# Windowed attention with sinks and two feed-forward layers: plain float32 products in place of split ones for the values and for the first batch's scores

## The chip, the cores and the metric

The kernel runs on one core of one Trainium2 chip. TensorE multiplies, VectorE (DVE), ScalarE (ACT) and GpSimd (POOL) work element by element, and SyncE (SP) issues nearly all transfers. The metric is device time in microseconds, the median of several executions: 657.28 us before the change (three runs, 656.28 to 657.93).

## What is computed

Attention for 2 batches, 8 heads, 768 positions and a head size of 64. A query sees its own and the 127 positions before it, and the first 4 positions (the sinks). Then come two feed-forward layers of 1536 tokens, model width 512 and hidden width 2048. All inputs and outputs are float32.

```python
scores = q @ k.T / sqrt(64)                      # masked to window 128 and 4 sinks
a = exp(scores - max); a = a / (sum(a) + 1e-9)
x = (a @ v).transpose(0, 2, 1, 3).reshape(1536, 512)
h = x @ w_in;   g = maximum(0.01 * h, h);  x = g @ w_out     # layer 1
h = x @ w2_in;  g = h * sigmoid(h);        y = g @ w2_out    # layer 2
```

## The kernel before

Each engine's program is written out by hand. All of them run over the same steps `a = 0..51` (`LAST = NPAIR + 4`). The queries are cut into 12 tiles `T` of 128 positions (6 to a batch); a tile has 4 pairs of heads, so that pair `u = 4T + p` is one of 48 and head `n` one of 96. Step `a` works on the scores of the next pair, the softmax of pair `a`, the transposes of pair `a-1` and the value products of pair `a-2`. A half `e` is two pairs: 4 heads of one tile.

The first `FS = 19` steps, called the head here, hold attention alone. From `a = 19` on each step also does one step `F = a - 19` of layer 1: `hidden(F+1)` (L1095, 12 products of 512 columns) and `project(F)` (L1112, another 12). Layer 1 has 48 such steps in three blocks of 512 tokens. `hidden(0)` needs `x` of tiles 0 to 3, so it waits for half 7. After attention, layer 1 runs on by itself, and then layer 2, whose first product is done by Strassen's scheme (`strassen`, L1139).

Every float32 operand of a matrix product is split in two parts of type fp32r: ACT writes the high part (a copy with a cast), and DVE or POOL writes the low part (the operand less the high part). A product then takes several passes of fp32r:

- Scores (`scores`, L1021): `q_st` holds the high part of q in partitions 0 to 63 and the low part in 64 to 127, `k_hl` the two parts of k, each in both halves of the partitions. Two passes of 260 columns (128 in the first tile of a batch) give a head's scores. ACT makes the high parts in `high_qk` (L548, two instructions for half a tile), POOL the low ones in `low_qk` (L434). So that both halves of the partitions have the data, `load_qk` (L321) loads it twice: 2 x 260 KB for half a tile.
- Values (`weigh_values`, L1062): stationary are 128 columns of v (two heads), moving are 256 columns of turned probabilities (two heads of 128 queries). For each of one or two key tiles three passes are run (`PASSES`). `high_v` (ACT, L559) and `low_v` (POOL, L456) split v; `high_pair` (ACT, L565) and `low_pair` (DVE, L761) copy the turned probabilities out of PSUM in two parts.
- The transposes of the probabilities (`turn_pair`, L1032) and of the inverse sums (`turn_half`, L1045), and the sink products (`weigh_sinks`, L1083).

In the head TensorE also runs filler products on zeros (`fill`, L1015): 24 ahead of everything, 3 in each of the steps 0 to 7, and 1 in each of the others. They give nothing to the result. The scores of the head go round three PSUM banks (`s_bank`), the transposes round two.

DVE's work for a step stands in this order: mask and maximum of two heads (`mask_max`, L748), `low_pair`, the sums' inverses, `take_half` or `scale_half` (L768, L796), then the low parts of first-layer weights (`low_win` L805, `low_wout` L811). SP issues in program order and waits in it: loads of q and k, of v, and from `a = 9` on the weights (`first_loads`, then `load_ws`).

Of the kernel before, what the change touches and what calls it, by code (L numbers as in the profile page):

```python
# [12 lines left out]
P = 128  # L13
# [4 lines left out]
def sink_window_attention_two_ffn(  # L18
    nc: bass.Bass, qk: bass.AP, vt: bass.AP, vsink: bass.AP, w1: bass.AP, w2: bass.AP, out: bass.AP,
    n_sink: int, window: int, seq: int,  # L20
):
    TILES, _, D, _, _ = qk.shape
    HD = vt.shape[2]
# [15 lines left out]
    NB = TILES // TB  # L39
    assert D == 64 and HD == 512 and REP == 4 and window <= P and NS <= P and FT == 16 and TILES == 12 and TPB == 6  # L40

    KEPT = 6
    RING = 4
    QR = 3

# [87 lines left out]
    with ExitStack() as ctx:  # L133
# [12 lines left out]
        w7_even_low = sb("w7_even_low", [P, 7, 2 * P], F32R)  # L146

# [9 lines left out]
        v_raw = sb("v_raw", [P, HD], F32)  # L157
        q_st = sb("q_st", [P, H, P], F32R)
        k_hl = sb("k_hl", [P, 2, H, PAN], F32R)
        v_hl = sb("v_hl", [P, 2, 2, HD], F32R)  # L160
# [17 lines left out]
        pT = sb("pT", [P, 2, 2, 512], F32R)  # L178
# [7 lines left out]
        def over(at, *tensors):  # L186
# [13 lines left out]
        (xs_even, w7_odd, w_sums, x_sums, w7_even_high), end = over(  # L200
            att_at, ("xs_even", [7, 2, BLK], F32R), ("w7_odd", [2, 7, 2 * P], F32R), ("w_sums", [2, 5, 2 * P], F32),
            ("x_sums", [2, 2 * P], F32), ("w7_even_high", [7, 2 * P], F32R))
# [18 lines left out]
        def o_bank(e):  # L221
            return y_ps[3] if e < E_EARLY and e % 2 else o_ps

# [32 lines left out]
        v_loaded = sem("v_loaded")  # L256
# [7 lines left out]
        v_high, v_ready = sem("v_high"), sem("v_ready")  # L264
# [8 lines left out]
        t_written, t_high, t_ready = sem("t_written"), sem("t_high"), sem("t_ready")  # L273
# [27 lines left out]
        def j_split(T):  # L301
            return 1 if T < TB else 3 if T == TB else 2

        split_1 = {(T, 3): T + 1 for T in range(TB)}
        split_1.update({(T, 0): T for T in range(TB + 1, TILES)})
# [14 lines left out]
        def _(sp):  # L320
            def load_qk(T, half):  # L321
                c = 2 * T + half
                wait(sp, k_ready, c - QR + 1)
                wait(sp, q_ready, c - QR + 1)
                for lo in (0, D):
                    sp.dma_start(qk_raw[lo:lo + D, c % QR, :, :], qk[T, half]).then_inc(qk_loaded[c % QR], 16)

            def load_v(T):
                wait(sp, v_ready, 2 * T)
                sp.dma_start(v_raw[:, :], vt[T]).then_inc(v_loaded, 16)  # L330
# [42 lines left out]
            load_qk(0, 0)  # L373
            load_qk(0, 1)
            load_v(0)
            load_qk(1, 0)
            for a in range(LAST):
                T, j = divmod(a, PAIRS)
                if j == 0 and T + 1 < TILES:
                    load_qk(T + 1, 1)  # L380
                if j == 2 and T + 1 < TILES:
                    load_v(T + 1)
                if j == 2 and T + 2 < TILES:
# [921 lines left out]
```

## Time and profile before

| | us |
|---|---|
| median of 3 runs | 657.28 |
| the profiled execution | 657.99 |
| its span, first to last instruction | 656.1 |
| `hidden(0)` begins (end of the head) | 65.2 |
| PE busy / DVE busy / ACT busy / POOL busy | 629.0 / 390.9 / 348.1 / 148.8 |

PE is TensorE's products, PEld its weight loads, which run beside the products. Rows of the time line merge neighbouring instructions of one kind, so a row's time covers all of its count; products overlap at their ends, so that the time from one to the next is less than the duration of one. In tables, "idle before" is the time that an engine stood still just before these instructions, and what ended it.

### The profile page before, as it was taken

How to read it: one execution, taken by the hardware profiler on the slowest of the kernel's cores; microseconds unless marked ns; L12 is line 12 of the kernel's file. 1: busy time of each engine (PE TensorE's matmuls, PEld its weight loads, DVE VectorE, ACT ScalarE, POOL GpSimd, SP SyncE). 2: the span in 40 equal slices, each digit the busy share in tenths (PEclk: the TensorE clock that was granted, in tenths of full speed). 3: DMA queues.
4: the chain of work that ended last, by engine and by line, in shares of the span. 5: the costliest groups of instructions: out<-in, count | busy, mean ns of one | idle time of the engine just before them, and what ended most of it. 6: DMA issues, size and time to landing. Idle time of an engine off the chain costs nothing.

```text
span 656.1 us, 10261 instructions
## 1 busy us (share of the span) xinstructions
PE 629.0 (96%) x3523; PEld 535.5 (82%) x3523; DVE 390.9 (60%) x812; ACT 348.1 (53%) x755; POOL 148.8 (23%) x181
## 2 busy tenths in 40 slices
PE   8896999989989999999999999999999999999997
PEld 4676787777878888888787888999998999999896
DVE  3887456555534656653157646676767677665652
ACT  6696656555545566642145446464655546454532
POOL 6775414232214323310418600000000000000000
PEclk9998999999999999999999999999999999999999
DMA  6666233334321232121148754434444543445401
GB/s 150 170 159 199 74 113 98 119 112 125 97 82 33 80 98 81 66 93 32 77 126 289 255 173 150 156 112 153 135 131 144 199 162 114 153 131 198 136 1 65
DMA packets 26611, 82.72 MB, mean 126 GB/s; under 512 B 3520, under 2 KB 3520, under 8 KB 26560
## 3 DMA queue, kind: packets, MB, share of 16 engines
q1 hardware_dynamic: 26176, 82.00, 39.7%
q8 instruction: 29, 0.48, 0.3%
q14 instruction: 22, 0.18, 0.1%
q10 hardware_dynamic: 384, 0.07, 0.1%
HBM read 73.66 MB, written 8.39 MB: 125 GB/s over the span
## 4 chain that ended last, share of the span: by engine, by line
PE 77%; DVE 9%; ACT 5%; issue 5%; POOL 1%; ACTq 0%; DVEq 0%; POOLq 0%
PE y_ps L1181 20%; PE h_ps L1106 18%; PE y_ps L1126 14%; PE s_ps L1134 8%; PE h_ps L1134 8%; PE t_ps L1134 3%; PE o_ps L1074 3%; DVE win L808 2%; DVE wout L814 2%; ACT prob L544 2%; PE t_ps L1042 1%; DVE g L819 1%; PE s_ps L1029 1%; ACT wout L587 1%; DVE att L802 1%
## 5 line engine op out<-in xcount | busy, mean ns | idle before, releaser
L1106 PE MATMUL h_ps<-x,win 128*128 128x512 f32 x576 | 144.7, 396 | 9.1 <-DVE win L808 5.2
L1126 PE MATMUL y_ps<-g,wout 128*128 128x512 f32 x576 | 146.9, 395 | 1.2 <-PE o_ps L1074 1.2
L1181 PE MATMUL y_ps<-wout,g 128*128 128x512 f32 x576 | 139.7, 391 | 0.0
L1106 PEld LDWEIGHTS h_ps<-x,win 128*128 128x128 f32 x576 | 104.7, 188 | 32.2 <-DVE win L808 6.9
L1181 PEld LDWEIGHTS y_ps<-wout,g 128*128 128x128 f32 x576 | 104.8, 188 | 20.4 <-issue 0.4
L1126 PEld LDWEIGHTS y_ps<-g,wout 128*128 128x128 f32 x576 | 103.6, 188 | 21.1 <-issue 2.3
L814 DVE TENSOR_TENSOR wout<-w_raw,wout 128x512 fp32r<-128x512 f32 x84 | 61.8, 736 | 59.4 <-ACT wout L587 59.4
L544 ACT ACTIVATE prob<-sm,neg_max 128x260 f32<-128x260 f32 (+1 forms) x96 | 47.0, 490 | 53.7 <-DVE neg_max L757 53.7
L593 ACT ACTIVATE g_f<-h_ps 128x512 f32<-128x512 f32 x48 | 28.6, 595 | 75.5 <-PE h_ps L1106 75.4
L650 ACT ACTIVATE g_f<-c_sum 128x512 f32<-128x512 f32 x24 | 15.2, 632 | 83.5 <-DVE c_sum L872 83.5
L819 DVE TENSOR_TENSOR g<-g_f,g 128x512 fp32r<-128x512 f32 x48 | 35.1, 732 | 30.1 <-ACT g L595 30.1
L587 ACT ACTIVATE wout<-w_raw 128x512 fp32r<-128x512 f32 x84 | 50.0, 623 | 0.0
L757 DVE CUSTOM_DVE_ANT_0 sm<-s_ps,mask 128x260 f32<-128x260 f32 (+1 forms) x71 | 28.7, 404 | 34.7 <-PE s_ps L1029 34.1
L461 POOL TENSOR_TENSOR v_hl<-v_raw,v_hl 128x256 fp32r<-128x256 f32 x24 | 20.4, 850 | 105.1 <-ACT v_hl L563 105.0
L879 DVE TENSOR_TENSOR g<-g_f,g 128x512 fp32r<-128x512 f32 x48 | 33.0, 687 | 17.6 <-ACT g L639 16.3
L446 POOL TENSOR_TENSOR q_st<-qk_raw,q_st 64x512 fp32r<-64x512 f32 x24 | 30.8, 1284 | 39.5 <-ACT q_st L555 37.9
L1134 PE MATMUL s_ps<-xs_even,w_odd 128*128 128x256 f32 x288 | 38.3, 282 | 0.0
L1134 PEld LDWEIGHTS s_ps<-xs_even,w_odd 128*128 128x128 f32 x288 | 37.2, 191 | 1.2
L1074 PE MATMUL o_ps<-pT,v_hl 128*128 128x256 f32 x222 | 34.6, 290 | 1.0 <-DVE pT L765 0.7
L1134 PE MATMUL h_ps<-xs_even,w_even_high 128*128 128x256 f32 x192 | 35.2, 282 | 0.0
L1029 PEld LDWEIGHTS s_ps<-k_hl,q_st 128*128 128x128 f32 x142 | 26.2, 190 | 9.9 <-issue 4.3
L1029 PE MATMUL s_ps<-k_hl,q_st 128*128 128x260 f32 (+1 forms) x142 | 29.8, 292 | 3.7 <-DVE neg_max L757 3.7
(133 smaller groups left out, 1017.3 us busy)
## 6 DMA issues: line engine op xcount, KB each, us to landing
w_sums<-w_sums SPq DMA_DIRECT2D x32, 640.0 KB, 3.9
w_raw<-w SPq DMA_DIRECT2D x36, 512.0 KB, 3.3
w_raw<-w SPq DMA_DIRECT2D x48, 384.0 KB, 3.0
qk_raw<-qk SPq DMA_DIRECT2D x48, 260.0 KB, 4.6
stage<-w SPq DMA_DIRECT2D x8, 512.0 KB, 5.3
v_raw<-vt SPq DMA_DIRECT2D x12, 256.0 KB, 2.9
y<-qk_raw SPq DMA_DIRECT2D x12, 256.0 KB, 3.8
vs_raw<-vsink ACTq DMA_DIRECT2D x8, 8.0 KB, 4.9
```

Of the source, the lines that this page charges most:

```text
L446: nc.gpsimd.tensor_tensor(q_low, qk_raw[D:P, c % QR, :, 0:P], q_low.bitcast(F32), ALU.subtract).then_inc(q_ready, 1)
L544: nc.scalar.activation(prob[:, n % PR, 0:W], sm[:, n % 2, 0:W], ACT.Exp, scale=-1.0, bias=neg_max[:, n % 4:n % 4 + 1], accum_out=row_sum[: ...
L587: nc.scalar.activation(wout[:, split_slot[j], 0, :], w_raw[:, j % RING, HD:2 * HD], ACT.Copy).then_inc(wout_high, 1)
L814: nc.vector.tensor_tensor(wout[:, slot, 1, :], w_raw[:, j % RING, HD:2 * HD], wout[:, slot, 0, :].bitcast(F32), ALU.subtract).then_inc(wou ...
L819: nc.vector.tensor_tensor(g[:, 1, F % 2, :], g_f32[:, F % 2, :], g[:, 0, F % 2, :].bitcast(F32), ALU.subtract).then_inc(g_ready, 1)
L879: nc.vector.tensor_tensor(g2[:, q % 2, 1, part, :], g_f32[:, half, :].rearrange("p (i n) -> p i n", i=2), g2[:, q % 2, 0, part, :].bitcast ...
L1029: ins = mm(bank_[:, 0:W], q_st[:, h, :], k_hl[:, part, h, 0:W], start=part == HI, stop=part == LO)
L1074: ins = mm(pair_out(u), v_hl[:, s, vp, p * P:(p + 1) * P], pT[:, u % 2, pp, s * 2 * P:(s + 1) * 2 * P], start=(u % 2 == 0 and s == 0 and v ...
L1106: ins = mm(h_ps[:, :], win[:, split_slot[split_of[F]], wp, c * P:(c + 1) * P], x[:, xp, c, tokens(F)], start=(c == 0 and wp == HI and xp = ...
L1126: ins = mm(y_ps[d][:, :], wout[:, split_slot[split_of[F]], wp, d * P:(d + 1) * P], g[:, gp, F % 2, :], start=(first and wp == HI and gp == ...
L1134: ins = mm(to, w_part(q, w_i, 1, wp)[:, 0, c * P:(c + 1) * P], x_part(q // FP, x_i, xp)[:, c, :], start=start and c == 0 and wp == HI and ...
L1181: ins = mm(y_ps[d][:, :], g2[:, q % 2, gp, at, d % 2 * P:(d % 2 + 1) * P], wout[:, slot, wp, :], start=(first and wp == HI and gp == HI), ...
```

## The change

- All value products (`weigh_values`) use v as loaded and the turned probabilities as copied, both plain float32, in one product for each key tile. `high_v`, `low_v` and `low_pair` go; `high_pair` becomes `take_pair`, one copy into a float32 `pT`. v has a ring of four tiles (`VR = 4`).
- The first batch's scores (tiles 0 to 5, `PLAIN = 6`) use q and k as loaded, in plain float32. Heads lie in partitions 0 to 63 or 64 to 127 (from a new input `qk_first`), and each tile is loaded once. A head's product contracts over 64 rows; outside the first tile it is two products, one of 132 and one of 128 columns (or 128 and 132), because the previous tile's keys are read where they were loaded. In the head the two heads of a pair alternate, product by product. `high_qk` and `low_qk` are left for tiles 6 to 11 only, at steps given by `split_0` and `split_1`.
- Filler: 6 in place of 24 at the start, and 1 in each step in place of 3 in the first eight.
- SP's order of loads follows this. Waits that counted pairs and halves together (`t_ready`) are now two semaphores. `w7_even_high` gets room of its own.

```diff
+            def load_plain(T):
+                wait(sp, s_written, H * (T - QR + 2) if T >= QR else 0)
+                raw = qk_raw[:, T % QR, :, :]
+                if T == 0:
+                    sp.dma_start(raw[:, 0:1, :], qk_first[T, :, 0:1, :]).then_inc(first_loaded, 16)
+                    sp.dma_start(raw[:, 1:, :], qk_first[T, :, 1:, :]).then_inc(plain_loaded[T % QR], 16)
+                else:
+                    sp.dma_start(raw, qk_first[T]).then_inc(plain_loaded[T % QR], 16)
...
             def load_v(T):
-                wait(sp, v_ready, 2 * T)
-                sp.dma_start(v_raw[:, :], vt[T]).then_inc(v_loaded, 16)
+                wait(sp, pv_done, PAIRS * (T - VR + 2) if T >= VR else 0)
+                sp.dma_start(v[:, T % VR, :], vt[T]).then_inc(v_loaded[T % VR], 16)
...
-                nc.scalar.activation(pT[:, u % 2, 0, 0:n], t_bank(k)[:, 0:n], ACT.Copy).then_inc(t_high, 1)
+                nc.scalar.activation(pT[:, u % 2, 0:n], t_bank(k)[:, 0:n], ACT.Copy).then_inc(pT_ready, 1)
...
-            def low_pair(u):
-                k = job["pair", u]
-                dve.wait_ge(t_high, u + 1)
-                n = 2 * P if width(u // PAIRS) == P else 4 * P
-                nc.vector.tensor_tensor(pT[:, u % 2, 1, 0:n], t_bank(k)[:, 0:n], pT[:, u % 2, 0, 0:n].bitcast(F32),
-                                        ALU.subtract).then_inc(t_ready, 1)
...
+            def plain_scores(heads):
+                T, W = heads[0] // H, width(heads[0] // H)
+                own = qk_raw[:, T % QR, :, :]
+                ahead = qk_raw[:, (T - 1) % QR, :, :]
...
+                for n in heads:
+                    wait(pe, s_read, freed(s_bank, n))
+                if W == P:
+                    parts = ((own, P, 0, P),)
+                elif T % 2:
+                    parts = ((own, P, P, P + NS), (ahead, P, 0, P))
+                else:
+                    parts = ((own, P, 0, P + NS), (ahead, P + NS, P + NS, P))
+                for part, (raw, at, to, size) in enumerate(parts):
+                    for n in heads:
+                        p, rows = n % H // 2, slice(n % 2 * D, (n % 2 + 1) * D)
+                        ins = mm(s_bank(n)[:, to:to + size], own[rows, p, 0:P], raw[rows, p, at:at + size],
+                                 start=part == 0, stop=True, skip_group_check=True)
...
-                    for vp, pp in PASSES:
-                        ins = mm(pair_out(u), v_hl[:, s, vp, p * P:(p + 1) * P],
-                                 pT[:, u % 2, pp, s * 2 * P:(s + 1) * 2 * P],
...
+                    tile = T if T % 2 == s else T - 1
+                    ins = mm(pair_out(u), v[:, tile % VR, p * P:(p + 1) * P],
+                             pT[:, u % 2, s * 2 * P:(s + 1) * 2 * P], start=u % 2 == 0 and s == 0,
+                             stop=only and s == slots[-1], skip_group_check=True)
...
-                        fill(24)
-                    for n in range(2 * a + 2 if a else 0, min(2 * a + 4, 2 * FS)):
-                        scores(n)
+                        fill(6)
+                    for n in range(2 * a + 2 if a else 0, min(2 * a + 4, 2 * FS), 2):
+                        plain_scores((n, n + 1))
...
-                    fill(3 if a < 2 * PAIRS else 1)
+                    fill(1)
```

## Rows read from the trace of the kernel before

**Rows 1.** The page's first part: busy time, share of the span, instructions.
```profile
PE 629.0 (96%) x3523; PEld 535.5 (82%) x3523; DVE 390.9 (60%) x812; ACT 348.1 (53%) x755; POOL 148.8 (23%) x181
```
**Rows 2.** Windows: length, busy (count) by engine, granted clock, DMA share, GB/s.
```profile
2.00:4.00 2.00, 2.00 (x6) 0.64 (x5) 0.00 (x0) 0.00 (x0) 1.77 (x6) 1.00 0.95 254
9.00:48.00 39.00, 33.68 (x224) 26.45 (x224) 32.22 (x117) 32.11 (x101) 30.56 (x35) 1.00 0.62 153
50.00:60.00 10.00, 7.32 (x46) 7.04 (x47) 7.77 (x26) 7.14 (x21) 5.49 (x7) 0.83 0.80 225
100.00:120.00 20.00, 18.97 (x102) 16.04 (x103) 11.55 (x32) 10.14 (x25) 6.61 (x8) 1.00 0.31 100
400.00:500.00 100.00, 100.00 (x632) 90.28 (x631) 69.99 (x111) 54.00 (x97) 0.00 (x0) 1.00 0.41 137
```
**Rows 3.** Time line of the start: start us, us, engine, line, tiles, count.
```profile
0.73 2.47 SPq L326 DMA_DIRECT2D qk_raw<-qk  x4
1.05 8.10 PE L1018 MATMUL y_ps<-filler 128*128 128x512 bf16 x24 [1.05 <-DVE filler L919]
...
5.12 1.28 ACT L555 ACT_TABLE_LOAD   x1 [5.12 <-issue]
...
10.02 0.40 ACT L544 ACTIVATE prob<-sm,neg_max 128x128 f32<-128x128 f32 x1
```
**Rows 4.** Time line of two steps of the head, ACT.
```profile
38.14 0.42 ACT L575 ACTIVATE x<-att 128x256 fp32r<-128x256 f32 x1 [0.59 <-DVE att L802]
38.46 0.58 ACT L570 ACTIVATE pT<-y_ps 128x512 fp32r<-128x512 f32 x1
38.94 0.50 ACT L544 ACTIVATE prob<-sm,neg_max 128x260 f32<-128x260 f32 x1
...
39.93 0.62 ACT L555 ACTIVATE q_st<-qk_raw 128x512 fp32r<-128x512 f32 x1
40.45 0.63 ACT L556 ACTIVATE k_hl<-qk_raw 128x528 fp32r<-128x528 f32 x1
...
41.75 0.42 ACT L563 ACTIVATE v_hl<-v_raw 128x256 fp32r<-128x256 f32 x1 [0.19 <-DMA v_raw<-vt]
...
43.38 0.42 ACT L575 ACTIVATE x<-att 128x256 fp32r<-128x256 f32 x1 [0.23 <-DVE att L802]
```
**Rows 5.** The same stretch, DVE.
```profile
39.07 0.69 DVE L765 TENSOR_TENSOR pT<-y_ps,pT 128x512 fp32r<-128x512 f32 x1 [0.15 <-ACT pT L570]
```
**Rows 6.** Time line of PE in the head.
```profile
19.37 0.82 PE L1018 MATMUL y_ps<-filler 128*128 128x512 bf16 x3
...
45.07 0.66 PE L1042 MATMUL t_ps<-ident,prob 128*128 128x128 f32 x4
...
46.97 0.40 PE L1029 MATMUL h_ps<-k_hl,q_st 128*128 128x260 f32 x2
...
51.03 0.77 PE L1029 MATMUL s_ps<-k_hl,q_st 128*128 128x260 f32 x2 [1.80 <-DVE neg_max L757]
...
65.20 2.97 PE L1106 MATMUL h_ps<-x,win 128*128 128x512 f32 x12 [0.58 <-POOL x L431]
```
**Rows 7.** Time line of PE and PEld in layer 1, beside attention.
```profile
104.22 0.87 PE L1074 MATMUL o_ps<-pT,v_hl 128*128 128x256 f32 x6
...
104.11 0.78 PEld L1074 LDWEIGHTS o_ps<-pT,v_hl 128*128 128x128 f32 x6
```
**Rows 8.** Groups by line and shape, 66 to 250 us: busy, mean ns, idle before.
```profile
L1074 PE MATMUL o_ps<-pT,v_hl 128*128 128x256 f32 x126 | 18.9, 283 | 0.3 <-DVE att L802 0.3
L1029 PEld LDWEIGHTS s_ps<-k_hl,q_st 128*128 128x128 f32 x92 | 17.1, 188 | 4.4 <-issue 0.8
...
L1042 PE MATMUL t_ps<-ident,prob 128*128 128x128 f32 x84 | 12.9, 272 | 0.1
```
**Rows 9.** Waits, 66 to 250 us: total us, times, longest.
```profile
PE h_ps L1106 <- DVE win L808: 5.2, 7, 1.4
```

More of the change, by code:

```diff
@@ L39, in sink_window_attention_two_ffn @@
     NB = TILES // TB
+    PLAIN = TPB
+    assert qk_first.shape[0] == PLAIN and qk.shape[0] == TILES - PLAIN
     assert D == 64 and HD == 512 and REP == 4 and window <= P and NS <= P and FT == 16 and TILES == 12 and TPB == 6
@@ L222, in o_bank, with early @@
             return y_ps[3] if e < E_EARLY and e % 2 else o_ps
+        def early(kind):
+            return sum(1 for (what, _), k in job.items() if what == kind and k < N_EARLY)
         def freed(bank_of, i):
@@ L255, in sink_window_attention_two_ffn @@
         qk_loaded = [sem(f"qk_loaded{i}") for i in range(QR)]
-        v_loaded = sem("v_loaded")
+        plain_loaded = [sem(f"plain_loaded{i}") for i in range(QR)]
+        first_loaded = sem("first_loaded")
+        v_loaded = [sem(f"v_loaded{i}") for i in range(VR)]
         vs_loaded = sem("vs_loaded")
@@ L299, in sunk @@
             return sum(has_sinks(s // 2) for s in range(e))
[L301 to L305, printed above, removed]
+        split_0 = {4 * T - 2: T for T in range(PLAIN, TILES)}
+        split_1 = {4 * T + (T == PLAIN): T for T in range(PLAIN, TILES)}
         CONSTS = 2 + 2 + 2 + 2 + 1 + 2
@@ L557, in high_qk, with take_pair @@
                                      ACT.Copy).then_inc(k_high, 1)
-            def high_v(T, half):
-                act.wait_ge(v_loaded, 16 * (T + 1))
-                wait(act, pv_done, PAIRS * (T - 1) + 2 * (half + 1))
-                part = slice(half * (HD // 2), (half + 1) * (HD // 2))
-                nc.scalar.activation(v_hl[:, T % TPB % 2, 0, part], v_raw[:, part], ACT.Copy).then_inc(v_high, 1)
-            def high_pair(u):
+            def take_pair(u):
                 k = job["pair", u]
@@ L682, in _ @@
                     high_x(scaled_in[a])
[L683 to L686 removed]
+                if a in split_1:
+                    high_qk(split_1[a], 1)
                 if a == FS:
[L688 removed]
                     take_hidden(0)
@@ L1030, in scores, with taken @@
                 ins.then_inc(s_written, 1)
+            def taken(before):
+                k = freed(t_bank, before) - 1
+                if k >= 0:
+                    what, i = list(job)[k]
+                    pe.wait_ge(pT_ready if what == "pair" else half_ready, i + 1)
             def turn_pair(u):
                 k = job["pair", u]
-                wait(pe, t_ready, freed(t_bank, k))
+                taken(k)
                 pe.wait_ge(exp_done, 2 * u + 2)
@@ L1046, in turn_half @@
                 k = job["half", e]
[L1047 removed]
+                taken(k)
                 pe.wait_ge(inv_spread, e + 1)
@@ L1119, in project @@
                         pe.wait_ge(s_read, S_TWO)
-                        pe.wait_ge(t_ready, N_EARLY)
+                        pe.wait_ge(pT_ready, early("pair"))
+                        pe.wait_ge(half_ready, early("half"))
                         pe.wait_ge(att_ready, E_EARLY)
```

149 lines of the change are left out of this document (66 added, 83 removed).

## The prediction

> **What bounds the kernel now.** I read the page's busy times first. PE is busy for 96% of the span [rows 1], so most of the time can only move if PE's work or its few pauses move. The table by windows then splits the span. In layer 2 (400 to 500 us) PE never stops [rows 2]; the change touches nothing there. Between 100 and 120 us, where attention runs inside layer 1, PE is busy 18.97 of 20 us [rows 2]: PE is still the limit, and each added pass costs its whole length. The head, up to the first product of `hidden(0)` at 65.2 us [rows 6], is different. From 9 to 48 us DVE, ACT and POOL are busy 32.2, 32.1 and 30.6 of 39 us, and PE's 33.7 us include fillers [rows 2]. No engine is full, they hand work round in a ring. The time line shows the period: ACT's copy of `x`, once for two steps, comes at 38.14 and 43.38 us [rows 4], so 5.24 us for two steps, 2.62 for one. After 48 us it is slower: 17 us for the last steps, where first-layer weights are split and where PE waited 1.80 us for DVE's maximum [rows 6], with the granted clock at 0.83 of full speed in the ten microseconds that follow (the level of 1.2 GHz for part of them) [rows 2].
>
> So I treat three stretches: the head (65.2 us), attention within layer 1, and the rest (unchanged).
>
> **What goes.** Of DVE: `low_pair`, 0.69 us for a wide pair [rows 5]. For two steps of the head that is 1.4 us, and DVE cannot be full in less than 5.24, so it keeps at most 3.9 us for two steps, 1.9 for one. Of ACT: in four steps it splits two halves of q and k (0.62 + 0.63 each) and two of v (0.42 each) [rows 4], 3.3 us, 0.8 a step. What stays is one copy of 0.58, two exponentials of 0.50 and half a copy of 0.42: 1.8 us. Of POOL: all the splits of q, k and v in the head; it is then no limit. So the element-wise engines would allow about 1.9 us a step in place of 2.62.
>
> The start moves too. Today the first exponential runs at 10.02 us [rows 3], behind two loads of both halves, ACT's two splits and those of DVE and POOL. After the change nothing lies between the load and the scores. ACT issues its own eight small transfers and loads its table until 6.4 us [rows 3], and this does not change, so the first exponential comes at about 6.5 us. Transfers run at 254 GB/s from 2 us on [rows 2], so the first pair of heads (133 KB) and the rest of the tile (400 KB) have landed before about 4.5 us. The six fillers left take 2 to 3 us (24 took 8.1 [rows 3]).
>
> **What PE pays.** No row before shows a plain float32 product that computes (the transposes only move data), so its price must be bounded. Two prices of PE are on record. Streaming: three fillers of 512 columns take 0.82 us, of which one is 0.38 long, so 0.215 us from one to the next [rows 6], or 0.107 for 256 columns. Weight loading: six weight loads of the value products take 0.78 us with 0.188 for a single one [rows 7, 8], so 0.118 from one to the next; that is also the pace of the six products themselves ((0.87 - 0.28) / 5 = 0.118) [rows 7, 8]. The cheapest that a float32 product can be is one pass, 0.118 us for 256 columns. The dearest that follows from the rows is all four products of two parts by two parts, one more than the three passes that the kernel spells out, each with a weight load of its own: 4 x 0.118 = 0.47 us. I take four streams at 0.107, 0.43 us, close to the upper end, because full precision wants the work of the three passes at the least (0.35), and the row nearest in kind is that of those passes.
>
> The Trainium skill, FP8 and Floating Point Precision, section TensorE Precision Notes, says that true float32 is four passes through the array; that would be this same 0.43. The Trainium skill, Perfetto Trace Analysis, section Engine Utilization, halves the output rate for the mode FP32_LOW_HIGH; were that the whole cost, a product would be 0.21 us. No row here shows either.
>
> A score product of 130 columns is by the same count 4 x 0.054 = 0.22 us when streaming sets the pace, and 4 x 0.115 = 0.46 us when every pass loads weights (the two passes of a head take 0.40 us and one is 0.285 long, so they stand 0.115 apart, the pace of weight loads again [rows 6]). The bounds are 0.115 (one pass) and 0.46. I take 0.22, and both ends stay in the range.
>
> **The head, summed.** PE's work up to `hidden(0)`: 38 heads, 8 with one score product and 30 with two, 68 x 0.22 = 15.0; transposes of 18 pairs, 4 x 2 + 14 x 4 = 64 at 0.12 ((0.66 - 0.27) / 3 is 0.13, a little less further on) [rows 6, 8] = 7.7; of 8 halves, 20 x 0.12 = 2.4; value products of 17 pairs, 4 + 13 x 2 = 30 x 0.43 = 12.9; sink products 8 x 0.12 = 1.0; 19 fillers x 0.215 = 4.1. Sum 43.1 us. The two heads of a pair use different halves of the array's rows and different banks. If they ran fully side by side, half of the 15.0 would go: 35.6. I take the middle, 39 us, 2.1 a step, just above what DVE and ACT allow. Ahead of it lie some 6 us (nothing but the first scores can run before the first exponential), and I allow 4.5 us for pauses: the weight splits in the last steps, which remain, and the last chain through DVE, ACT and POOL that `hidden(0)` waits for. That puts `hidden(0)` at 50 us, 15 earlier than now. Transfers do not stop it: up to there five tiles of q, k and v (0.79 MB each), a sixth on its way and four weights of 0.5 MB are about 7 MB, 30 us at 225 to 254 GB/s [rows 2].
>
> **Attention within layer 1.** Here PE is the limit and pays in full. 27 wide pairs: 2 x 0.43 in place of 6 x 0.12, +0.14 each, 3.8 us. Four pairs of tile 6 with one key tile: 0.43 for 0.36, 0.3 us. Ten heads of tiles 4 and 5 still have plain scores, one head at a time: 0.44 in place of 0.22 (two passes 0.115 apart), 2.2 us. Together +6.3. On the other side PE waits seven times, 5.2 us in all, for DVE's low part of `win` [rows 9]. DVE loses 0.69 us a step, which stands ahead of that split in DVE's order, but the wait also runs through ACT, which is not relieved as much in this stretch. I count half, 2.5 us. Net +3.8. The new waits of SP (a free v slot, scores of a tile done before its buffer is loaded again) stand ahead of weight loads in its queue. The one that is latest, for the scores of tile 5 at `a = 24`, is met within the step before, while its data are wanted one to two steps of 5.7 us later; I count nothing for it, and up to 1 us if the cover fails.
>
> Span: 656.1 - 15 + 3.8 = 644.9. The profiled execution took 1.9 us more than its span and lies 0.7 above the median, so **646 us**.
>
> **Rivals.**
> 1. Rows of the array side by side. If the two heads of a pair overlap fully, 3.5 us more go from the head, and with fewer pauses and all of the 5.2 us regained it is 638. For it: different row halves and banks, in alternation. Against: DVE and ACT then bind at 1.9 us a step.
> 2. Emptying the array at each change of shape. Scores contract over 64 rows and everything between them over 128. If PE must finish all before it changes, each change costs the tail of a product: one is 0.28 long at 0.118 apart [rows 7, 8], so some 0.17. Two changes in each of 19 steps are 6.5 us, and 20 in layer 1 3.4 us more: 656, no change worth the name. The Trainium skill, TensorEngine Tiling (Array Packing), section Key Properties, says that changing the tiling mode drains the engine; this speaks against the change, and no row before has a product of 64 rows.
> 3. The other side: every pass loads its weights. A score product then costs 0.46 and a value product 0.47. The head is 43.1 + 68 x 0.24 + 30 x 0.04 = 60.6 us with no overlap, 71 with start and pauses, and layer 1 pays 10 x 0.69 + 27 x 0.23 = 13.1 for 2.5 regained: 656.1 + 6 + 10.6 = 672.7, measured 674. It turns into a loss from about 0.31 us a score product on: there the head gains only 6 us and layer 1 costs as much. Weight loads busy 82% of the span today [rows 1] speak for it; that only 2 parts of a weight exist speaks against it.
> 4. The clock. With 24 fillers cut to 6 and 3 to 1, PE idles after its first scores until the first exponential. Before, a pause of 1.80 us at 51 us [rows 6] stands beside 0.83 of the clock over the next ten [rows 2]. Were the lower level held through the head, streams double: 68 x 0.43 + 30 x 0.86 + 8.2 of filler + the 11 us that loads set = 74 us, `hidden(0)` at 85; with the 3.8 of layer 1 the span is 680, measured 681. It turns into a loss from some 25 us at the lower level.
> 5. The head is shorter but the gain is eaten by the transfers: weights and tiles pulled into a shorter time, as at 50 to 60 us now, with 0.80 of the DMA engines busy [rows 2]. Then `hidden(0)` comes at 58 or so: 654.
>
> **How the numbers follow.** Chances: forecast 0.52 (640 to 652), rival 1 0.14, rival 2 0.12, rival 3 0.10, rival 4 0.05, rival 5 0.07. The range 634 to 660 holds the forecast, rivals 1, 2 and 5, and leaves the two losses of rivals 3 and 4 out, apart from milder forms of them. A measurement of this kernel can tell 0.3% (2 us) from no change. Faster: forecast, rival 1, most of rival 5 and some of rival 2, 0.76. Same: 0.08. Slower: rivals 3 and 4 and a little of 2, 0.16.
>
> **What will show it.** Right: `hidden(0)` near 50 us; first exponential near 6.5; 0.43 us from one value product to the next; PE above DVE in the head; in layer 1 PE busy more and its waits for `win` down; nothing moved from the end of attention on. Wrong: 0.45 us for a score product or weight loads that fill the head (rival 3); gaps around each block of scores (rival 2); a granted clock near half in the head (rival 4); PE waiting for tiles or weights (rival 5). The weakest term is the price of a plain float32 product, for which no row stands.

## The result, and the profile after

The changed kernel takes 653.33 us (median of 5, 652.15 to 654.31) against 657.29 for the kernel before it, run beside it: a ratio of 0.9936, 95% interval [0.9917, 0.9954]. That is 4.0 us less. 11.3 were forecast, so the sign and the range held, and the size did not.

The first lines to set beside [rows 1] and [rows 2]: busy times, then the windows of the same stretches (columns as in [rows 2]).

```profile
PE 632.4 (97%) x3481; PEld 532.4 (82%) x3481; DVE 358.9 (55%) x762; ACT 330.2 (51%) x707; POOL 102.2 (16%) x135
...
9.00:48.00 39.00, 36.88 (x257) 26.68 (x257) 26.53 (x106) 25.81 (x83) 8.77 (x18) 1.00 0.33 113
50.00:60.00 10.00, 8.26 (x50) 6.60 (x50) 4.38 (x18) 4.82 (x15) 1.30 (x3) 1.00 0.24 81
100.00:120.00 20.00, 20.00 (x103) 16.77 (x103) 10.11 (x30) 11.01 (x29) 4.30 (x6) 1.00 0.66 176
400.00:500.00 100.00, 100.00 (x633) 90.53 (x632) 72.49 (x117) 56.11 (x101) 0.00 (x0) 1.00 0.41 135
```

From 9 to 48 us DVE, ACT and POOL fall from 32.2, 32.1 and 30.6 us to 26.5, 25.8 and 8.8, while PE rises from 33.7 to 36.9 of 39. PE is now the bound of the head, as foreseen. The engines that were relieved bring nothing more.

The time line of PE in one whole period of the head (two steps) shows what it does with that time.

```profile
35.01 0.38 PE L1017 MATMUL y_ps<-qk_raw 64*128 64x132 f32 x1
35.02 0.38 PE L1017 MATMUL s_ps<-qk_raw 64*128 64x132 f32 x1
35.23 0.27 PE L1017 MATMUL y_ps<-qk_raw 64*128 64x132 f32 x1
...
35.45 0.27 PE L1017 MATMUL s_ps<-qk_raw 64*128 64x128 f32 x1
35.66 0.66 PE L1054 MATMUL t_ps<-ident,prob 128*128 128x128 f32 x4
36.15 1.03 PE L1086 MATMUL y_ps<-pT,v 128*128 128x256 f32 x4
37.01 0.38 PE L993 MATMUL y_ps<-filler 128*128 128x512 bf16 x1
37.32 0.38 PE L1017 MATMUL h_ps<-qk_raw 64*128 64x132 f32 x1
...
40.22 0.38 PE L1017 MATMUL s_ps<-qk_raw 64*128 64x132 f32 x1
...
50.67 0.35 PE L1017 MATMUL s_ps<-qk_raw 64*128 64x132 f32 x1 [1.57 <-DVE neg_max L751]
...
56.87 3.01 PE L1117 MATMUL h_ps<-x,win 128*128 128x512 f32 x12 [1.07 <-POOL x L458]
```

Three readings. A plain product shows as two records: the four of a wide pair of value products stand (1.03 - 0.38) / 3 = 0.215 us apart, so a product is 0.43 us, the forecast price exactly. The two heads of a pair truly run side by side: their records start 0.01 us apart. And around the block stand gaps. The block's last record begins at 35.45, and the transposes begin 0.21 later, where records inside the block are 0.11 apart; the block's first record, too, is followed only after 0.22. The filler at 37.01 is followed by the scores after 0.31 in place of 0.215. Two steps take 5.21 us (35.01 to 40.22). The 5.24 of [rows 4] is not typical of the kernel before: from the transposes of one half's inverse sums to those of the next it took 4.4 to 7.5 us in the head, 42.6 from half 0 to half 7, where the changed kernel takes 38.3. `hidden(0)` begins at 56.87 us in place of 65.20 [rows 6], 8.3 earlier; 50 was forecast. Of the 8.3, 3.5 are there when half 0 is turned, that is when its inverse sums are transposed (13.04 against 16.52), 4.3 come between half 0 and half 7, and 0.5 after it.

So 8.3 us were gained by the end of the head, and 5.3 are left in the span (656.1 to 650.8). Where the rest went shows in the transposes of the inverse sums, one for each half, in the same place in both programs. In half 8, the first within layer 1, the changed kernel leads by 8.3 us (59.48 against 67.78, by their weight loads), in half 11 by 5.3, in half 19 by 4.8 and in half 23 by 3.9. Three microseconds go within the few steps that still score tiles 4 and 5; one goes slowly from half 19 on, 0.14 a step, the forecast extra cost of a wide pair. Later, between 345 and 360 us, the kernel before loses 1.4 us that the changed one doesn't, 0.92 of it in one pause at 359.58. `one_head` and `early_fill` below have that pause and `changed_again` lacks it, with no difference between their programs there, so I credit it to neither.

### The profile page after: what moved, and what is told of

It reads as the page before. It is cut to its first block, busy times and chain, and to the rows that moved or that the text cites. A ratio compares the mean times of both kernels' runs of the same rounds, so it can differ in the third digit from the quotient of the medians.

```text
span 650.8 us, 9903 instructions
## 1 busy us (share of the span) xinstructions
PE 632.4 (97%) x3481; PEld 532.4 (82%) x3481; DVE 358.9 (55%) x762; ACT 330.2 (51%) x707; POOL 102.2 (16%) x135
## 4 chain that ended last, share of the span: by engine, by line
PE 92%; DVE 3%; issue 2%; ACT 2%; ACTq 1%; POOL 0%; DVEq 0%
PE y_ps L1194 20%; PE h_ps L1117 20%; PE y_ps L1138 19%; PE h_ps L1146 8%; PE s_ps L1146 8%; PE o_ps L1086 5%; PE t_ps L1146 3%; PE t_ps L1054 2%; PE s_ps L1034 1%; PE s_ps L1017 1%; PE t_ps L1064 1%; DVE win L795 1%; ACTq L668 1%; PE y_ps L1086 1%; PE y_ps L1017 1%
## 5 line engine op out<-in xcount | busy, mean ns | idle before, releaser
L1138 PE MATMUL y_ps<-g,wout 128*128 128x512 f32 x576 | 151.6, 403 | 1.2 <-PE o_ps L1086 1.2
L1138 PEld LDWEIGHTS y_ps<-g,wout 128*128 128x128 f32 x576 | 105.6, 188 | 22.9 <-issue 2.7
L801 DVE TENSOR_TENSOR wout<-w_raw,wout 128x512 fp32r<-128x512 f32 x84 | 60.4, 720 | 57.0 <-ACT wout L590 57.0
L1086 PE MATMUL o_ps<-pT,v 128*128 128x256 f32 x148 | 39.7, 388 | 0.3 <-DVE att L789 0.3
L1146 PE MATMUL s_ps<-xs_even,w_odd 128*128 128x256 f32 x288 | 38.3, 282 | 0.0
L449 POOL COPY inv_wide<-row_inv 128x256 f32<-128x256 f32 x24 | 10.0, 417 | 154.6 <-DVE row_inv L781 154.6
L795 DVE TENSOR_TENSOR win<-w_raw,win 128x512 fp32r<-128x512 f32 x36 | 31.4, 871 | 1.4 <-ACT win L584 1.3
L1146 PEld LDWEIGHTS h_ps<-xs_even,w_even_high 128*128 128x128 f32 x192 | 30.3, 188 | 1.6 <-DVE e_sum L853 0.3
L573 ACT ACTIVATE pT<-t_ps 128x512 f32<-128x512 f32 (+1 forms) x40 | 22.5, 562 | 17.4 <-PE t_ps L1054 17.4
```

The costliest lines, as they stand in the source:

```text
L795: nc.vector.tensor_tensor(win[:, slot, 1, :], w_raw[:, j % RING, 0:HD], win[:, slot, 0, :].bitcast(F32), ALU.subtract).then_inc(win_ready, 1)
L801: nc.vector.tensor_tensor(wout[:, slot, 1, :], w_raw[:, j % RING, HD:2 * HD], wout[:, slot, 0, :].bitcast(F32), ALU.subtract).then_inc(wou ...
L1086: ins = mm(pair_out(u), v[:, tile % VR, p * P:(p + 1) * P], pT[:, u % 2, s * 2 * P:(s + 1) * 2 * P], start=u % 2 == 0 and s == 0, stop=onl ...
L1138: ins = mm(y_ps[d][:, :], wout[:, split_slot[split_of[F]], wp, d * P:(d + 1) * P], g[:, gp, F % 2, :], start=(first and wp == HI and gp == ...
L1146: ins = mm(to, w_part(q, w_i, 1, wp)[:, 0, c * P:(c + 1) * P], x_part(q // FP, x_i, xp)[:, c, :], start=start and c == 0 and wp == HI and ...
```

## The experiments

**Each half of the change alone.** `values_only` is the kernel before with the value half; `scores_only` is the changed kernel without it; `old_fills` has both halves and the fillers of before.

```diff
  values_only: scores, their loads and fillers as before
-                    for vp, pp in PASSES:
+                    tile = T if T % 2 == s else T - 1
+                    ins = mm(pair_out(u), v[:, tile % VR, p * P:(p + 1) * P],
+                             pT[:, u % 2, s * 2 * P:(s + 1) * 2 * P], ...)
```

> The kernel before with the value half of the change alone (plain float32 values, one copy of the turned probabilities; scores and fillers as before). Theory A, the head was bound by VectorE's 4.9 us in 5.24: without the low parts it needs 3.5, ScalarE 4.4, GpSimd 3.9 plus its waits, and TensorE 4.6 to 4.7 for two steps. So 4.7 in place of 5.24, hidden(0) at about 61 us; layer 1 costs 0.14 us a step more on TensorE (4.1) and gets 2.5 back; total near 654.5. Theory B, TensorE alone decides everywhere: the head stays, total 3 us slower than before, 660.

It takes 649.28 us against 657.01 for the kernel before beside it, 7.7 us less and more than the whole change brings (ratio 0.9898 [0.9878, 0.9919]). `hidden(0)` begins at 57.39. The same two steps of the head, from the transposes of one half to those of the next but one:

```profile
34.87 0.38 PE L1033 MATMUL t_ps<-ident,inv_wide 128*128 128x128 f32 x2
...
35.20 0.60 PE L1023 MATMUL y_ps<-ident,prob 128*128 128x128 f32 x4
35.63 1.03 PE L1055 MATMUL o_ps<-pT,v 128*128 128x256 f32 x4
36.40 0.50 PE L1071 MATMUL o_ps<-psT,vs_st 128*128 128x256 f32 x2
...
36.78 0.59 PE L1003 MATMUL y_ps<-k_hl,q_st 128*128 128x260 f32 x2
37.21 0.40 PE L1003 MATMUL s_ps<-k_hl,q_st 128*128 128x260 f32 x2
37.45 0.60 PE L1023 MATMUL t_ps<-ident,prob 128*128 128x128 f32 x4
...
39.45 0.38 PE L1033 MATMUL y_ps<-ident,inv_wide 128*128 128x128 f32 x2
```

4.58 us for two steps, with PE again without a pause, against 5.21 with plain scores. Theory A's 4.7 is met, but not its totals: 61 us for `hidden(0)` and 654.5 were expected, because the sum took 5.24 for every two steps of the kernel before, where most took longer. DVE, ACT and POOL are busy for 3.5, 4.3 and 4.0 us of the 4.58. The edit takes splits of v off ACT and POOL along with DVE's low parts, so that it frees the ring as a whole; no run frees DVE alone. From half 8 to half 23 this kernel takes 234.65 us; the kernel before takes 234.10: the float32 values cost 0.55 us there, not 1.6. A wide pair does cost its 0.14 us, but PE stands still for 6.9 us of the stretch in place of 9.2; the waits for `win` among it are 3.8 us in place of the 5.2 of [rows 9]. That layer 1 hides so much of PE's extra work I had counted only in part.

```diff
  scores_only: the changed kernel, with values, weights and their waits as before
-                    ins = mm(pair_out(u), v[:, tile % VR, p * P:(p + 1) * P], ...)
+                    for vp, pp in PASSES:
+                        ins = mm(pair_out(u), v_hl[:, s, vp, p * P:(p + 1) * P],
+                                 pT[:, u % 2, pp, s * 2 * P:(s + 1) * 2 * P], ...)
```

> The changed kernel with the value half undone (values and turned probabilities in two parts again, three passes). Start and fillers as in the changed kernel. Theory A: VectorE has its low parts back and two steps need 5.2 us on it and on TensorE alike, so that the head gains only at its start, hidden(0) at about 61 us; layer 1 pays 0.27 us for the changes of shape and 0.22 us for streaming in each of ten heads, 4 to 5 us, against no gain later on; total near 657. Theory B, splitting q and k was what held the head: hidden(0) at 57 as in the changed kernel, total 652.

653.22 us, ratio 0.9946 [0.9928, 0.9965]; `hidden(0)` at 59.84. Between the two expectations. Two steps take 5.28 us there (33.22 to 38.50), with PE busy for 5.15 and DVE for 4.80: DVE's low parts and PE's plain scores need about the same time. Of the 5.4 us by which `hidden(0)` comes earlier than before, 3.9 are there when half 0 is turned (12.61 us) and 1.5 come between half 0 and half 7; from half 8 to half 23 it loses 2.1 us, not 4 to 5.

```diff
  old_fills: the changed kernel, with
-                        fill(6)
+                        fill(24)
-                    fill(1)
+                    fill(3 if a < 2 * PAIRS else 1)
```

> The changed kernel with the fillers of the kernel before (24, and 3 in each of the first eight steps). The 24 fillers end at 9.1 us, 2.7 us after ScalarE could take the first exponential, and 16 more fillers cost 0.215 us each where TensorE is the bound, 3.4 us; the clock is at its upper level from 6.5 us on, which gave 2.4 us in early_fill. Theory A: hidden(0) at about 56.87 + 2.7 + 2.2 - 2.4 = 59.4 us, total 2 us slower than the changed kernel. Theory B (fillers are free as they were before): hidden(0) at 56 or less.

656.36 us, ratio 0.9997 [0.9986, 1.0008], `hidden(0)` at 59.09: theory A, though not by its own working, since the 24 fillers ended at 7.7 us and not at 9.1 (the clock came up earlier in this execution). These runs together make the sum of the change. The value half brings 7.7 us. The plain scores, added to it with the fillers unchanged, take 7.1 back (649.28 to 656.36). Fewer fillers bring 3.0 (656.36 to 653.33). The kernel before ran beside each group of runs, with medians of 657.0 to 657.6; by the ratios to it the three parts are 6.7, 6.5 and 4.0 us, so each is known to about 1 us. The traces show where they lie:

| us | half 0 is turned at | half 0 to half 7 | half 8 to half 23 |
|---|---|---|---|
| before | 16.5 | 42.6 | 234.1 |
| `values_only` | 15.9 | 36.0 | 234.6 |
| `scores_only` | 12.6 | 41.1 | 236.2 |
| `old_fills` | 13.9 | 39.6 | 238.3 |
| changed | 13.0 | 38.3 | 238.5 |

Plain scores start the head earlier (no split lies between the load and the scores), and cost more in each step after that than the start gives.

**What plain scores cost.** In `full_rows` each score product contracts over all 128 rows, that is over both heads of a pair, so its scores are sums of two heads' and stand for nothing but their time. The heads can't run side by side, and the array's shape never changes.

```diff
-                        p, rows = n % H // 2, slice(n % 2 * D, (n % 2 + 1) * D)
+                        p, rows = n % H // 2, slice(0, P)
```

> The changed kernel with score products that contract over all 128 rows (both heads of a pair at once, so the scores are sums of two heads' and not the reference's). No side by side is possible, but the shape of the array never changes. Theory A, a change of shape costs about 0.16 us: 38 changes in the head go, 6 us, against 7.5 us for the lost overlap, hidden(0) at about 58; and in layer 1 the step from single plain scores gets 0.3 us cheaper per head. If changes of shape cost nothing: hidden(0) at about 64, as with one head after the other.

One execution, 651.89 us, `hidden(0)` at 57.36. Its start is 1.0 us earlier than the changed kernel's (half 0 at 12.06), with part of its first products short; from half 0 to `hidden(0)` it takes 45.3 us against 43.8, the 1.5 more that theory A expects. Two steps of the head:

```profile
34.63 0.46 PE L1017 MATMUL y_ps<-qk_raw 128*128 128x132 f32 x2
34.93 0.39 PE L1017 MATMUL s_ps<-qk_raw 128*128 128x132 f32 x2
35.15 0.38 PE L1017 MATMUL y_ps<-qk_raw 128*128 128x128 f32 x2
35.37 0.39 PE L1017 MATMUL s_ps<-qk_raw 128*128 128x128 f32 x2
35.59 0.60 PE L1054 MATMUL t_ps<-ident,prob 128*128 128x128 f32 x4
...
40.11 0.46 PE L1017 MATMUL s_ps<-qk_raw 128*128 128x132 f32 x2
```

A product of 130 columns is 0.22 us, as forecast. Two steps take 5.48 us, only 0.27 more than the changed kernel, although the overlap, 4 x 0.22 = 0.88 us, is gone. So 0.61 us came back for the four changes of shape that are gone: 0.15 us each. In layer 1 the same shows alone, since a head comes singly there and has no overlap to lose: from half 8 to half 23 `full_rows` takes 235.71 us, the changed kernel 238.46. Nine heads with plain scores lie in between, so 2.75 us is 0.15 for each of their eighteen changes. The Trainium skill, TensorEngine Tiling (Array Packing), section Key Properties, says that a change of tiling mode drains the engine; the trace agrees, with 0.15 us a change here and 0.2 in the single step below.

Within layer 1, the same step of the changed kernel, of `full_rows` and of `values_only` (split scores):

```profile
79.23 1.64 PE L1117 MATMUL h_ps<-x,win 128*128 128x512 f32 x6
80.80 0.71 PE L1017 MATMUL s_ps<-qk_raw 64*128 64x132 f32 x4
81.44 1.13 PE L1086 MATMUL o_ps<-pT,v 128*128 128x256 f32 x4
82.22 1.74 PE L1138 MATMUL y_ps<-g,wout 128*128 128x512 f32 x6
```
```profile
78.46 1.64 PE L1117 MATMUL h_ps<-x,win 128*128 128x512 f32 x6
...
81.06 1.73 PE L1138 MATMUL y_ps<-g,wout 128*128 128x512 f32 x6
```
```profile
78.12 1.64 PE L1086 MATMUL h_ps<-x,win 128*128 128x512 f32 x6
79.59 0.41 PE L1003 MATMUL s_ps<-k_hl,q_st 128*128 128x260 f32 x2
79.84 1.03 PE L1055 MATMUL o_ps<-pT,v 128*128 128x256 f32 x4
80.51 1.73 PE L1107 MATMUL y_ps<-g,wout 128*128 128x512 f32 x6
```

From the start of the six products to that of the value products it is 2.21 us in the first against 1.72 in the last, and to the next six, by which time the second change has been paid as well, 2.99 against 2.39: 0.60 more for one head, of which 0.22 was forecast. `full_rows` needs 2.60. So the two changes of shape are 0.39 of the 0.60, 0.2 each; over the whole stretch shorter waits for `win` give part of that back.

**Side by side or not.** `one_head` issues all products of a head before those of the next.

```diff
-                    for n in range(2 * a + 2 if a else 0, min(2 * a + 4, 2 * FS), 2):
-                        plain_scores((n, n + 1))
+                    for n in range(2 * a + 2 if a else 0, min(2 * a + 4, 2 * FS)):
+                        plain_scores((n,))
```

> The changed kernel with the two heads of a pair one after the other in the head, not product by product in turn. If the two halves of the array's rows truly work side by side, this loses it: a pair of score products of 0.44 us becomes two, 15 steps x 0.44 + 4 x 0.22 = 7.5 us more, hidden(0) at about 64 us. If the records only look simultaneous: hidden(0) stays at 56.9.

One execution, 653.8 us, `hidden(0)` at 56.51: nothing is lost. This does not refute the overlap, since its own time line shows it:

```profile
34.71 0.38 PE L1017 MATMUL y_ps<-qk_raw 64*128 64x132 f32 x1
34.73 0.38 PE L1017 MATMUL s_ps<-qk_raw 64*128 64x132 f32 x1
34.93 0.27 PE L1017 MATMUL y_ps<-qk_raw 64*128 64x132 f32 x1
34.94 0.27 PE L1017 MATMUL s_ps<-qk_raw 64*128 64x132 f32 x1
```

The second head (`s_ps`) starts 0.02 us after the first although it is issued behind all of it. The experiment could not take the overlap away; `full_rows` did.

**The fillers and the clock.** `no_late_fill` drops the fillers from step 4 on; `early_fill` has 3 in steps 0 to 2.

```diff
  no_late_fill
-                    fill(1)
+                    fill(1 if a < 4 else 0)
  early_fill
-                    fill(1)
+                    fill(3 if a < 3 else 1)
```

> The changed kernel without the fillers of steps 4 to 18 (15 of them). Theory A, TensorE is the bound in the head: in the changed kernel two steps take 5.21 us and TensorE has no pause in them, so each filler costs its 0.215 us. Of 15 fillers, two stand just before a pause for a maximum and save nothing; 13 x 0.215 = 2.8 us less, hidden(0) at about 54.1 in place of 56.9 us, total near 650.5. Theory B, the ring through VectorE and ScalarE is the bound and TensorE only looks full: less than 0.5 us of change. A third outcome, the granted clock falls without fillers: later than 56.9.

652.27 us, ratio 0.9924 [0.9907, 0.9942]; `hidden(0)` at 56.19, 0.7 earlier. The scores at 34 to 39 us come about 1 us earlier (4.90 us for two steps in place of 5.21, so some 0.155 for each filler), but the stretch 35 to 57 us then shows 0.92 of the clock, where the changed kernel shows 1.00:

```profile
35.00:57.00 22.00, 18.13 (x119) 14.54 (x118) 13.70 (x51) 14.11 (x41) 4.84 (x12) 0.92 0.25 88
```

Both theory A, at less than its price, and the third outcome are in it. That the missing fillers brought the clock down is likely and not shown: it is one execution of each, and the kernel before, with its fillers, shows 0.92 in the same stretch too.

> The changed kernel with 3 fillers in place of 1 in steps 0 to 2, so that TensorE does not stand still between the first scores and the first transposes. Theory A (the low clock at the start costs time): in the changed kernel a filler after 6 us is still 0.63 us long and only one at 14.6 us is 0.38; here the short ones should begin before 11 us, and the scores of heads 10 and 11, at 15.0 us, come at about 13.5; total 1 to 1.5 us less. Theory B (the chain from scores through maximum, exponential and transpose sets the pace of the first steps): the scores of heads 10 and 11 stay at 15.0 or come later by the added fillers.

652.25 us, ratio 0.9924 [0.9908, 0.9941]; `hidden(0)` at 54.47. It can't be credited to the added fillers: products were short from 5.3 us on, before the first of them ran. What the run does show is the price of the lower level. Heads 10 and 11 are scored at 12.65 us there and at 15.03 in the changed kernel, whose fillers at 6.01, 8.68 and 11.31 us are still 0.61 to 0.63 long (at that length they stand 0.43 us apart, at 0.38 long 0.215: the levels of 1.2 and 2.4 GHz).

```profile
15.03 0.35 PE L1017 MATMUL h_ps<-qk_raw 64*128 64x132 f32 x1
```
```profile
12.65 0.35 PE L1017 MATMUL h_ps<-qk_raw 64*128 64x132 f32 x1
```

(First the changed kernel, then `early_fill`.) Not all of these 2.4 us is the clock. The first exponential stands right behind ACT's own small transfers and its table load, and these let it start at 5.88 us in `early_fill` and at 6.39 in the changed kernel. From it to heads 10 and 11 it is 6.77 us against 8.64: 1.9 for the lower level.

`changed_again` is the changed kernel once more, and `warm_start` has 12 fillers ahead and 3 in steps 0 to 2.

```diff
  warm_start: early_fill, with
-                        fill(6)
+                        fill(12)
```

> The changed kernel itself once more, for the moment at which TensorE's products become short. It was about 14 us in its first profile, 12.7 in no_late_fill (same start), 9.5 and 5.0 in early_exp and early_fill (which have the same TensorE program). Theory A, the moment varies from execution to execution and moves the whole head: a different moment here, and the scores of heads 10 and 11 (15.0 before) follow it with about half of the shift; hidden(0) anywhere from 54.5 to 57. Theory B, it is set by the program: 14 us again, hidden(0) at 56.9.

> The changed kernel with 12 fillers at the start, which end at about 6.2 us, and 3 in steps 0 to 2. In the kernel before, 24 fillers in a row brought the products to their short length at 6.3 us. Theory A: here too, in every execution, and although the first scores wait until 6.2 us (3.7 before), heads 10 and 11 are scored at about 13.5 in place of 15.0, hidden(0) at about 55.4, total near 652 and with a smaller spread. Theory B, the chain decides: the later first scores push everything back by 1.2 us or more, total 654.5.

`changed_again` takes 652.89 us, 0.9934 [0.9918, 0.9951], with products long until some 14 us and `hidden(0)` at 56.62 (8.72 us from the first exponential to heads 10 and 11): theory B for this program, in the two executions that were profiled. `warm_start` takes 652.42, 0.9925 [0.9909, 0.9941], `hidden(0)` at 56.07; its products are short from the first scores on, but these come 2.6 us later, and heads 10 and 11 follow at 14.24, 6.98 us behind its first exponential. Theory A's 13.5 and 55.4 are missed by 0.7.

```profile
6.01 0.61 PE L993 MATMUL y_ps<-filler 128*128 128x512 bf16 x1
...
11.07 0.63 PE L993 MATMUL y_ps<-filler 128*128 128x512 bf16 x1
...
14.56 0.38 PE L993 MATMUL y_ps<-filler 128*128 128x512 bf16 x1
```
```profile
2.73 3.62 PE L993 MATMUL y_ps<-filler 128*128 128x512 bf16 x8
6.29 0.37 PE L1017 MATMUL s_ps<-qk_raw 64*128 64x128 f32 x1
```

(First `changed_again`, then `warm_start`, whose row holds the last 8 of the 12 fillers.) The lower level at the start costs about 1.9 us (8.64 less 6.77); a start that avoids it by fillers gives most of that back by being late. The totals of the changed kernel, `early_fill` and `warm_start` (653.3, 652.3, 652.4) are no further apart than their spreads.

`early_exp` is `early_fill` with the loads of the sinks' values issued by SP, behind its first loads, instead of by ACT ahead of its exponentials.

```diff
  early_exp: early_fill, with, in the SP queue ahead of its loop (and gone from ACT's)
+            for b in range(B):
+                for r in range(REP):
+                    n = H * NS
+                    sp.dma_start(vs_raw[r * n:(r + 1) * n, b, :], vsink[b]).then_inc(vs_loaded, 16)
```

> The changed kernel with 3 fillers in steps 0 to 2 (as in the run early_fill) and, new, the eight small loads of sink values issued by SyncE behind its first loads in place of ScalarE. ScalarE then loads its table from 0.7 us on, and the first exponential waits for the mask alone (4.7 us on GpSimd) and VectorE's first maximum: at about 5.4 us in place of 6.39. Theory A (the first steps are a chain through this exponential): hidden(0) 0.7 to 1 us earlier than in early_fill, 53.5 to 53.8. Theory B (TensorE's work sets it): no change, 54.5.

Its first exponential comes at 5.17 us, but it takes 652.25 us in all, 0.9928 [0.9906, 0.9949], and `hidden(0)` at 55.87: later than in `early_fill`, since its products are long until some 9.3 us. An earlier exponential and a lower clock meet in this run, so it leaves the question open. That the first exponential is a link of the chain shows in the traces (first the changed kernel, then `early_exp`):

```profile
7.03 0.29 DVE L751 CUSTOM_DVE_ANT_0 sm<-y_ps,mask 128x128 f32<-128x128 f32 x1 [1.68 <-ACT prob L553]
7.47 0.55 PE L1017 MATMUL h_ps<-qk_raw 64*128 64x128 f32 x1 [0.85 <-DVE neg_max L751]
```
```profile
6.08 0.29 DVE L751 CUSTOM_DVE_ANT_0 sm<-y_ps,mask 128x128 f32<-128x128 f32 x1 [0.73 <-PE s_ps L1017]
```

In the changed kernel the third head's maximum waits 1.68 us for the first exponential, and PE's next scores wait 0.85 us for that maximum. In `early_exp` the same maximum waits for PE's scores, which run at the lower level.

**A version to beat both.** Two more kernels start from `values_only`; the second also has the edit of `early_exp`.

```diff
  values_few_fills
-                        fill(24)
+                        fill(14)
-                    fill(3 if a < 2 * PAIRS else 1)
+                    fill(3 if a < 3 else 1)
  values_early_table
-                        fill(24)
+                        fill(8)
-                    fill(3 if a < 2 * PAIRS else 1)
+                    fill(3 if a < 3 else 1)
```

> The kernel with the value half alone (as in the run values_only), with 14 fillers at the start in place of 24, 3 in steps 0 to 2 and 1 in the others. The first scores wait for VectorE until 9.09 us anyway, so the first ten are free to drop as long as the clock stays up; in steps 3 to 7, ten fillers go. Theory A, TensorE is the bound of the head here too (4.57 us for two steps): 10 x 0.215 = 2.1 us less at most, hidden(0) at about 55.5, total 647.5. Theory B, ScalarE and GpSimd pace the first steps: within 0.5 us of values_only.

651.83 us, ratio 0.9913 [0.9896, 0.993], `hidden(0)` at 58.88, 1.5 us later than in `values_only`: neither expectation. The total is 2.5 us above that of `values_only`, though the two intervals overlap. The first ten fillers dropped were not free:

```profile
5.00:10.00 5.00, 2.41 (x11) 1.29 (x9) 1.49 (x2) 3.61 (x5) 2.57 (x2) 0.90 1.02 239
10.00:15.00 5.00, 5.00 (x20) 3.66 (x20) 2.43 (x15) 3.96 (x15) 2.10 (x3) 0.50 0.92 234
```
```profile
9.08 0.69 PE L1003 MATMUL s_ps<-k_hl,q_st 128*128 128x128 f32 x2 [2.59 <-DVE k_hl L901]
```

PE stands still for 2.6 us before the first scores, and the granted clock from 10 to 15 us is 0.50. The halves 0 to 4 then follow each other as in `values_only` (18.95 us against 18.96), so the ten fillers of steps 3 to 7 cost nothing there.

> As values_few_fills, with 8 fillers at the start and the eight small loads of sink values issued by SyncE behind its first loads instead of by ScalarE. In values_only ScalarE issues them until 5.1 us and loads its table until 6.4, and only then splits q and k. Here the table is loaded by about 2 us and the first split waits for the data alone, about 4 us. Theory A, this chain sets the start: the first scores come at about 7 in place of 9.1 us, hidden(0) 1.5 to 2 us earlier than in values_few_fills, total 645.5 to 646. Theory B, the clock comes up later because TensorE has less to do at the start: part of it is lost, 647.

649.82 us, ratio 0.9879 [0.9864, 0.9894], `hidden(0)` at 57.34: almost 3 us above the nearer of the two expectations. The first scores come at 8.14 us in place of 9.09, but half 0 is turned at 15.78 in place of 15.92: what the earlier start gained, the clock took (its fillers at 9.91 us are still long). It ties with `values_only`. Both are faster than the changed kernel: the interval of this one lies clear of its [0.9917, 0.9954], and the executions of `values_only` (649.3 to 651.6 us) lie below all of its own (652.2 to 654.3). The simplest version to keep is the value half with the old scores and the old fillers, 649.3 us.

## Why the prediction was right or wrong

The mechanism was right: the ring of the element-wise engines bound the head, float32 values free it, PE takes over, and layer 1 pays. (That DVE was the tightest of them is argued from its order of work; no run freed it alone.) The prices of single products, 0.43 and 0.22 us, were met to the hundredth. The size was wrong by 7.3 us. The step that failed is the head's sum: 50 us forecast for `hidden(0)`, 56.9 measured. It took half of the overlap of the scores where all of it is there, and had no term for the changes of shape, for the lower clock at the start and for the chain of the first steps.

- **The first four steps**, 4.3 us. By the forecast's own prices steps 0 to 3 are 4.7 us of PE work (12 score products half side by side, 8 transposes, 2 value products, 4 fillers) behind 6 us of start, so heads 10 and 11 are due at 10.7; they came at 15.0. The first exponential, at 6.4, is 0.4 of this, and 1.9 is the lower clock. I had named it as rival 4 with a chance of 0.05 and only as a thing of the whole head; it comes in a mild form, in nearly every run whose fillers stop early, and in the likeliest case it should have been a term. The other 2.0 us are there with the products short as well (6.77 from the first exponential in `early_fill`, for the same 4.7 of work and some fillers): with three pairs in flight each step is a chain from scores over maximum and exponential to transposes, and a sum of PE's work alone has no term for that. No run took this chain apart.
- **From there to `hidden(0)`**, 2.7 us: 41.8 measured, where the sum leaves 39.1. The pauses were met, 4.6 us for the 4.5 allowed. The middle between full overlap and none was the wrong form: the overlap is full (rival 1), and each change of shape costs 0.15 us (rival 2, priced at 0.17). Rivals that touch the same instructions can hold at once. In these 14 blocks of scores the full overlap gives 3.1 us more than the middle, and 28 changes take 4.3, so 1.2 net. Another 0.7 is head 38, which is scored ahead of `hidden(0)` (55.09 us) and which the forecast's 38 heads, 0 to 37, left out. Some 0.7 stays open. For two steps the prices add up to 0.88 + 0.96 + 0.36 + 1.72 + 0.24 + 0.43 = 4.59 us with full overlap, and to 5.47 with none; `full_rows`, without overlap and without changes, measured 5.48. The 0.62 from 4.59 to the 5.21 of the changed kernel are its four changes.
- **Layer 1**, +4.4 us from half 8 to half 23 where +3.8 was forecast. A near hit made of two misses: the values cost 0.55 and not 1.6, the heads with plain scores 3.8 and not 2.2, the difference being their changes of shape.
- **Not in the forecast at all**: the scores' half is a loss once the values' half is in. By the forecast's own figures this could have been seen: a pair of split scores was 4 x 0.115 = 0.46 us on PE, a plain pair 0.44 at its very best, and splitting q and k loaded only ACT and POOL, which are not what binds the head once DVE is free (4.3 and 4.0 of 4.58 us in `values_only`). The forecast summed the change as one and never asked each half for its price.
- Rival 3 (weights loaded for every pass) fell: a product of 130 columns would be 0.46. Rival 5 (transfers) fell: from 9 to 48 us the DMA engines are 0.33 busy, 0.62 before [rows 2], and from 50 to 60 us 0.24, 0.80 before. That its numbers, `hidden(0)` at 58 and 654 us, are near the measured ones is luck. Rival 4's price was too low by its own mechanism: it left the transposes at their old pace, but at the lower level they stand 0.21 us apart in `changed_again` (13.28 and 13.49 us), 0.11 at the upper.

## What to carry to other kernels

Price each half of a change separately, at the engine that will bind once the other half has worked; here one half gave some 7 us and the other took nearly as much back. Halving the rows of the array for small products pays only if the overlap gained between two changes of shape exceeds their price, here 0.44 us for a pair against 0.30 to 0.4, and nothing when heads come singly. Work that keeps TensorE busy while it has nothing to do is part of the start: see what the granted clock does before dropping it.

## What the runs showed of the hardware

- Plain float32 products of 256 columns stand as two records 0.215 us apart: 0.43 us a product at the upper clock level, four times the 0.107 us that 256 columns of a filler take.
- Products in different halves of the array's rows run side by side even when one head's are all issued before the other's (0.02 us apart in `one_head`).
- A change between 64 and 128 rows costs 0.15 to 0.2 us (5.48 against 5.21 us for two steps with four changes and 0.88 us of overlap; 2.75 us for eighteen changes in layer 1; 2.99 against 2.60 us for two changes in one step of it).
- The same TensorE program can see its products become short at 5.3 us in one execution and at some 9.3 in another (`early_fill`, `early_exp`). Even 24 fillers in a row, begun at 1.05 us, became short at 3.9 us in `old_fills`, 5.3 in `values_only` and 6.6 in the kernel before. In the changed kernel it was between 13 and 14 us twice. In `full_rows` products were short at 4.0 us, long again from 7.5 to 10.5 and short from 10.9 on. What sets the moment stays open. The profile's clock column shows 1.00 for the changed kernel's start, although its fillers are 0.63 us long there: at the start of a trace the durations are to be trusted before that column.
